# A second PSUM bank for the down sums, a fourth early expert visit, a late table in two parts, and a reordered start, in a fused attention and two-layer MoE kernel

## The reference, cut to what matters

```python
# 1. linear attention with decay: batch 4, heads 8, sequence 768, head size 48
for t in range(S):
    cur = einsum('bhd,bhe->bhde', u[None] * kt, vt)
    y[:, :, t] = einsum('bhd,bhde->bhe', rt, state + cur)
    state = wt[:, :, :, None] * state + einsum('bhd,bhe->bhde', kt, vt)
# 2. gated layer on 3072 tokens of 384 (d_ff 1024)
x = (((x @ w1) * (x @ w2)) @ w3) @ w_out
# 3. top-2 of 8 experts, noisy gate, expert d_ff 1024
noisy = x @ w_gate + log1p(exp(x @ w_noise)) * noise
top2, weights = two largest of noisy, softmax of the two
out[token] += weight * (relu(x[token] @ ew1[e]) @ ew2[e])
```

## Time and profile before

| | us |
|---|---|
| median of 3 runs | 1050.75 (1049.59, 1050.75, 1053.85) |
| the profiled execution's own time | 1053.97 |
| its span, first to last instruction | 1052.2 |
| PE busy | 1013.2 (96% of the span) |
| DVE / ACT / POOL busy | 705.6 / 584.3 / 221.7 |
| DMA | 166.41 MB, mean 158 GB/s |

### The profile page before, as it was taken

The page is one execution under the profiler, slowest core; times in us unless marked ns, Lnnn a source line. Parts: engine busy times, 40 slices in busy tenths (PEclk is TensorE's granted clock), DMA queues, the critical chain, the costliest instruction groups (busy, mean ns, idle before and its releaser), DMA issues.

```text
span 1052.2 us, 20504 instructions
## 1 busy us (share of the span) xinstructions
PE 1013.2 (96%) x7769; PEld 951.2 (90%) x7769; DVE 705.6 (67%) x1339; ACT 584.3 (56%) x1126; POOL 221.7 (21%) x210
## 2 busy tenths in 40 slices
PE   5999999999999989999998999999999999999995
PEld 3666799989999989999998999999999999999995
DVE  4789567788778767735677567575765857476570
ACT  4555446546556536533473556575665756567471
POOL 0000000110110110111313332443333234333421
PEclk9999999999999999999999999999999999999998
DMA  9564432453544542120657979787887978778761
GB/s 258 148 157 109 104 68 63 86 127 67 77 86 110 96 45 44 43 87 16 231 93 125 283 202 301 208 262 219 240 256 217 300 212 247 245 225 269 226 158 16
DMA packets 190887, 166.41 MB, mean 158 GB/s; under 512 B 118259, under 2 KB 174453, under 8 KB 190789
## 3 DMA queue, kind: packets, MB, share of 16 engines
q1 hardware_dynamic: 177012, 144.76, 49.9%
q0 software_dynamic: 12976, 20.32, 9.8%
q10 hardware_dynamic: 800, 0.02, 0.0%
HBM read 141.21 MB, written 25.22 MB: 158 GB/s over the span
## 4 chain that ended last, share of the span: by engine, by line
PE 90%; DVE 4%; ACT 2%; SPq 2%; issue 1%; DMA 0%; POOL 0%; another core or an unknown queue 0%; DVEq 0%; ACTq 0%; POOLq 0%
PE pp L1222 19%; PE bank L1206 19%; PE bank L797 19%; PE fx L813 9%; PE tr L162 3%; PE yu L1265 3%; PE fx L695 2%; PE pp L177 2%; PE yu L223 2%; PE bank L695 2%; PE yu L217 2%; PE tr L1187 2%; PE yu L1247 1%; PE fx L1247 1%; PE yu L198 1%
## 5 line engine op out<-in xcount | busy, mean ns | idle before, releaser
L797 PE MATMUL bank<-xh,w12h 128*128 128x256 f32 x576 | 167.8, 291 | 1.7 <-DVE ab_all L875 1.1
L797 PE MATMUL bank<-xl,w12h 128*128 128x256 f32 x576 | 163.5, 284 | 0.0
L797 PE MATMUL bank<-xh,w12l 128*128 128x256 f32 x576 | 163.4, 284 | 0.0
L1120 POOL DMA_INDIRECT result<-x2s,who x55 | 93.4, 1699 | 276.2 <-ACT x2s L1339 260.7
L1326 DVE SCALAR_TENSOR_TENSOR abl<-bank,abh 128x512 fp32r<-128x512 f32 x96 | 66.2, 690 | 110.7 <-ACT abh L1321 101.6
L975 POOL DMA_INDIRECT slot_entry<-entry,slot_i x48 | 48.4, 1009 | 377.3 <-DVE token_f L964 366.1
L797 PEld LDWEIGHTS bank<-xh,w12h 128*128 128x128 f32 x576 | 110.8, 192 | 4.5 <-DVE ab_all L875 2.0
L797 PEld LDWEIGHTS bank<-xl,w12h 128*128 128x128 f32 x576 | 110.9, 193 | 0.0
L797 PEld LDWEIGHTS bank<-xh,w12l 128*128 128x128 f32 x576 | 110.8, 192 | 0.0
L1206 PE MATMUL bank<-xh,set_up_h 128*128 128x256 f32 x384 | 109.2, 284 | 0.0
L1206 PE MATMUL bank<-xl,set_up_h 128*128 128x256 f32 x384 | 108.6, 283 | 0.0
(11 more groups left out here) (237 smaller groups left out, 2750.2 us busy)
## 6 DMA issues: line engine op xcount, KB each, us to landing
up_raw<-in_moe_w SPq DMA_DIRECT2D x93, 512.0 KB
down_raw<-in_moe_w SPq DMA_DIRECT2D x124, 384.0 KB
padded<-in_w SPq DMA_DIRECT2D x32, 144.0 KB, 3.1
padded<-in_k SPq DMA_DIRECT2D x32, 144.0 KB
padded<-in_r SPq DMA_DIRECT2D x32, 144.0 KB
vs<-in_v SPq DMA_DIRECT2D x32, 144.0 KB, 3.1
attention_out<-yt SPq DMA_DIRECT2D x64, 72.0 KB, 1.9
xr<-attention_out SPq DMA_DIRECT2D x12, 384.0 KB, 3.7
```

Of the source, the lines that this page charges most:

```text
L797: last = nc.tensor.matmul(bank[f % 2][:, m * TG:(m + 1) * TG], wp[:, m, kk, f * P:(f + 1) * P], xp[:, kk, :], start=(n == 0), stop=(n == 3 ...
L1120: nc.gpsimd.indirect_dma_start(out, bass.IndirectOffsetOnAxis(who[v % 4][:, s, 0:1], 0), yo[v % 2][:, s, 0:DM], None, bounds_check=N - 1, ...
```

## The change

1. `pair_slots` takes `first`: while pair 0 runs, the `diag` steps of pair 1 stand in slots 3, 4 and 5 instead of 0, 1 and 4, its `spread` steps in 6, 7, 8, 9 instead of 5, 6, 8, 9. The turns of `w_out`, the gates and the first turn of `w3` are dealt over the slots before pair 0 alone (`front`); everything from the first `w3_mm` on comes from pair 0 on. A half of the next `w3_turn` stands behind the second and fourth quarter instead of ahead of the first and third. The split of `w1`, `w2` is one block later. SP loads `w3` block 1 ahead of the second pair's w, k, r, and `w1` piece 0 behind them.
2. `pe_down` sums the second half in `bank[1]`; it waits for `fx_free` only ahead of the first half. `up` step 1 of the next group (and `hidden` step 1 of visit 0) waits for the copy out of `bank[1]`.
3. The last `place` goes to `fx` and no longer waits for `h_free`.
4. `EARLY` is 4 and `BIG` is 20; the small visits stay 5, 9, ..., 29. The late table is made in two parts: 16 instructions where all 26 stood, and the last 10 between the two `lower` halves of visit 1.
5. In the middle SP waits, after each store of `x2s`, each zeroing of `result` and each load of `xr`, until that DMA has landed, before it goes on.

```diff
-EARLY, BIG, SMALL = 3, 21, 7
+EARLY, BIG, SMALL = 4, 20, 7
...
-            for part, at in enumerate(SPREAD_AT[q]):
+            for part, at in enumerate((3, 4, 5) if first else (0, 1, 4)):
+                slots[at].append(("diag", q + 1, part))
+            for part, at in enumerate((6, 7, 8, 9) if first else SPREAD_AT[q]):
                 slots[at].append(("spread", q + 1, part))
...
             for n in range(KF):
                 for quarter in range(4):
-                    if quarter % 2 == 0 and n + 1 < KF:
+                    build.append(("w3_mm", n, quarter))
+                    if quarter % 2 and n + 1 < KF:
                         build.append(("w3_turn", n + 1, quarter // 2))
-                    build.append(("w3_mm", n, quarter))
-            order = threaded(build, first_slots() + [slot for q in range(HP) for slot in pair_slots(q)] + [[]] * TAIL)
+            order = threaded(front, first_slots())
+            order += threaded(build, [slot for q in range(HP) for slot in pair_slots(q, q == 0)] + [[]] * TAIL)
...
-                load_w12(0)
+                load_w3(1)
                 for n in range(3):
                     sp_input_load(sp, 0, 1, n)
-                load_w3(1)
+                load_w12(0)
...
-                if f == 1 and i == 0:
-                    pe.wait_ge(wal_ready, KF)
+                if f == 1:
+                    need(pe, fx_free, 2 * i)
+                    if i == 0:
+                        pe.wait_ge(wal_ready, KF)
...
-                if third == 0:
+                if third == 0 and s == 0:
                     need(pe, fx_free, fx_down(b, q, s))
...
-                        last = nc.tensor.matmul(fx[:, 0:WA], xp[:, f, s * P:(s + 1) * P], wp[:, f, :],
+                        last = nc.tensor.matmul(sum_at[s][:, 0:WA], xp[:, f, s * P:(s + 1) * P], wp[:, f, :],
...
                 if i == NG * B - 1:
-                    pe.wait_ge(h_free, 3)
+                    pe.wait_ge(fx_free, 2 * NG * B - 1)
...
+                    if j == 1:
+                        finale.append(("late", 1, 1))
                     finale.append(("lower", j, 1))
...
                             sp_group_store(sp, b, q)
+                            sp.wait_ge(x2_stored[q], 16 * (b + 1))
                         elif (step, q, n) == ("down", NG - 1, 3):
                             sp.wait_ge(fx_free, fx_down(b, q, 0) + 1)
                             sp_group_load(sp, b + 1, NG - 1)
+                            sp.wait_ge(xr_loaded[NG - 1], 16 * (b + 2))
...
                                 sp_clear(sp, HP * b + q)
+                                sp.wait_ge(zeros_stored, 16 * (HP * b + q + 1))
```

More of the change, by code:

```diff
@@ L362, in program, with pair_slots @@
         SPREAD_AT = ((5, 6, 8, 9), (5, 7, 8, 9), (5, 6, 7, 9), (6, 7, 8, 9))
[L364 to L367 removed]
+        def pair_slots(q, first=False):
+            slots = [[("score", q, 0), ("keys", q, 0)],
+                     [("score", q, 1), ("state", q, 0)],
                      [("in", q + 1, 0), ("scale", q, 0)],
                      [("in", q + 1, 1), ("derive", q + 1, 0)],
[L370 removed]
+                     [("out", q, 0), ("derive", q + 1, 1)],
                      [("out", q, 1), ("in", q + 1, 2), ("derive", q + 1, 2)],
                      [("derive", q + 1, 3)], [("derive", q + 1, 4), ("derive", q + 1, 5)], [], []]
[L373 removed]
+            for part, at in enumerate((3, 4, 5) if first else (0, 1, 4)):
+                slots[at].append(("diag", q + 1, part))
+            for part, at in enumerate((6, 7, 8, 9) if first else SPREAD_AT[q]):
                 slots[at].append(("spread", q + 1, part))
@@ L544, in first_sp @@
                         load_w3(q + 2)
-                    elif step == "w3_mm" and n == 3 and q + 2 < 6:
-                        load_w12(q + 2)
+                    elif step == "w3_mm" and n == 3 and 1 <= q < 2 * KD - 1:
+                        load_w12(q + 1)
                     elif step == "score" or step == "in" and q:
@@ L588, in first_act @@
                         evacuate(6 + 2 * q + n)
[L589 to L593, removed]
+                    elif step == "w3_mm" and n == 1 and 1 <= q <= 2 * KD:
+                        m, kk = divmod(q - 1, KD)
+                        act.wait_ge(wraw_loaded[(q - 1) % 2], 16 * ((q - 1) // 2 + 1))
+                        nc.scalar.copy(w12h[:, m, kk, :], wraw[(q - 1) % 2][:, :]).then_inc(w12h_ready, 1)
                     elif step == "w3_mm" and n == 3:
@@ L635, in first_dve @@
                                               ).then_inc(wo_ready, 1)
[L636 to L640, removed]
+                    elif step == "w3_mm" and n == 2 and 1 <= q <= 2 * KD:
+                        m, kk = divmod(q - 1, KD)
+                        dve.wait_ge(w12h_ready, q)
+                        nc.vector.tensor_tensor(w12l[:, m, kk, :], wraw[(q - 1) % 2][:, :], w12h[:, m, kk, :].bitcast(f32),
                                                 ALU.subtract).then_inc(w12l_ready, 1)
@@ L755, in fx_down, with place_at @@
                 return 2 * i + s
-            place_at = bank[0][:, 0:ST * E]
+            sum_at = (fx, bank[1])
+            def place_at(i):
+                return (fx if i == NG * B - 1 else bank[0])[:, 0:ST * E]
             CLEARS = HP * (B - 1)
@@ L852, in act_down @@
                     act.wait_ge(fx_full, fx_down(b, q, s) + 1)
-                    nc.scalar.copy(x2s[q][:, s, :], fx[:, 0:WA]).then_inc(fx_free, 1)
+                    nc.scalar.copy(x2s[q][:, s, :], sum_at[s][:, 0:WA]).then_inc(fx_free, 1)
             def act_route(act, b, q, part):
@@ L1045, in program @@
             GROUPS = NG * B
-            small = [v >= EARLY and (v - EARLY) % 4 == 2 for v in range(NV)]
+            small = [v >= EARLY and (v - EARLY) % 4 == 1 for v in range(NV)]
             slot = [BIG + sum(small[:v]) if small[v] else v - EARLY - sum(small[:v]) for v in range(NV)]
@@ L1197, in pe_hidden @@
                         pe.wait_ge(ab_free, KF * GROUPS)
-                if v < 2 and m == 0:
-                    pe.wait_ge(place_free, GROUPS - 1 + v)
+                if v == 0 and m == 0:
+                    pe.wait_ge(place_free, GROUPS - 1)
+                if v == 0 and m == 1:
+                    pe.wait_ge(fx_free, 2 * GROUPS)
                 need(pe, h_free, 4 * bigs(v) + m - 1)
@@ L1471, in rest_sp @@
                 sp_group_store(sp, B - 1, 2)
-                sp_weights(sp, 2)
+                for v in range(2, EARLY):
+                    sp_weights(sp, v)
                 for v in range(EARLY, NV):
@@ L1618, in rest_pe @@
                         pe_count(pe, GROUPS - NG)
-                    elif step == "late":
+                    elif step == "late" and n == 0:
                         pe_count(pe, GROUPS)
```

78 lines of the change are left out of this document (41 added, 37 removed).

## The result

The changed kernel takes 1046.2 us (median of 20 runs, 1038.4 to 1052.7); the kernel before, in the same comparison, 1053.3 us (20 runs, 1047.7 to 1055.6). The ratio is 0.9945, 95% interval 0.9929 to 0.9961, a gain of 5.8 us (the medians differ by 7.1). The forecast was 1037.9 us with a range up to 1043.0, so the result lies outside. In two later comparisons, in which the kernel before took 1063.1 and 1056.4 us, the changed kernel stood at 0.9945 (0.9918 to 0.9972) and 0.9992 (0.9965 to 1.0019).

A forecast was written before the change was run, and what follows sets the result against it. PE work is 90% of the chain of waits, so only closing PE holes or raising its clock saves time. 6.8 + 4.3 + 0.6 + 0 + 4.4 = 16.1 us off 1053.97 gives 1037.9 us; range 1033.4 to 1043.0.

The forecast's parts named there:

- Part 1: At the start: first scores come 9.95 us earlier, 3.13 us of work still owed; gain 6.8 us, bounds 4.0 to 7.3.
- the 18.9 us that I took: At the start: time of the first scores after the change, straight behind the gates and waiting for DVE alone.
- Parts 2 and 3: Second bank ends eight waits for the copy out of fx, 4.3 us; last place starts earlier, 0.6 us.
- Part 4: Fourth early visit, late table in two, around visit 1's hidden: gain 0; 2.5 us if ACT's lateness was chance.
- over 10 us to spare: Slack claimed for visit 4's gather, though SP reads that visit's table some 3 us later than before.
- the 1.81 us for which DVE waited for ACT: At visit 1's first hidden step, behind the late table: taken to show that removing the table alone brings nothing.
- Part 5: In the middle: SP's waits for landings remove a 3.4 us hole and 1.0 us of slow clock; 4.4 us, bounds 0 to 5.1.
- my first rival: In the middle: slow mixture stays, part 5 brings nothing, parts 1 to 3 work; 1042.3 us, chance 0.22.
- the 3.2 us between the profiled execution and the median: Whole kernel: the median lies 3.2 us below the profiled execution, whose stall was read as occurring only in some executions.
- 12.9 us: Whole kernel: forecast gain counted from the median instead of the profiled execution, 1.2%.
- some 13: End of the kernel: time without PE work behind the last matmul, in us, which the change does not touch.

The follow-up runs named there:

- e12: Kernel before with part 1 of the change alone; ratio to the kernel before 0.9931 (0.9907 to 0.9956).
- e17: Kernel before with parts 2 and 3 of the change alone; 1046.5 against 1051.4 us, ratio 0.9956 (0.9940 to 0.9972).
- e3: Kernel before with part 5 of the change alone; ratio to the kernel before 0.9997 (0.9976 to 1.0019).
- e9: The changed kernel itself, timed again in a later comparison; ratio to the kernel before 0.9945 (0.9918 to 0.9972).
- e13: The changed kernel itself, timed again in another later comparison; ratio to the kernel before 0.9992 (0.9965 to 1.0019).
- e15: Changed kernel without part 4, timed beside the changed kernel on one chip; ratio to the kernel before 0.9937 (0.9911 to 0.9964).
- e7: Changed kernel without part 4 (three early visits, late table in one piece); ratio to the kernel before 0.9879 (0.9842 to 0.9916).
- e11: Changed kernel without part 4, third visit's gather moved ahead of the last group's scatters; ratio to the kernel before 0.9889 (0.9856 to 0.9921).
- e16: Changed kernel with the third visit's gather ahead of the last group's scatters, beside the changed kernel on one chip; ratio to before 0.9839 (0.9815 to 0.9863).
- e1: Changed kernel without part 5's four SP waits; ratio to the kernel before 0.9933 (0.9908 to 0.9958).
- e2: Changed kernel, each group's x2s store held until the scatters of all groups before it have landed; ratio to the kernel before 0.9938 (0.9916 to 0.9960).
- e5: Changed kernel with the third visit's gather ahead of the last group's scatters; 1040.0 against 1057.1 us before, ratio 0.9829 (0.9804 to 0.9854).
- e18: Changed kernel with the edits of e2 and e5 together; 1033.0 us, ratio to the kernel before 0.9826 (0.9806 to 0.9845).
- e14: Changed kernel, fourth visit's weights held until the third visit's gather has landed; ratio to the kernel before 0.9941 (0.9914 to 0.9969).
- e4: Changed kernel without part 5's SP waits, each store held until earlier groups' scatters have landed; ratio to the kernel before 0.9929 (0.9908 to 0.9951).

## Why the prediction was wrong, by its own steps

**Part 1, forecast 6.8 us: right.** The first `up` came at 107.75 where 107.5 was forecast (106.6 to 110.2 over all profiles with part 1), and e12 measured 7.3 us (interval 4.7 to 9.8) at the end of the kernel. The clock stayed at 1.00 up to the first `up`. The scores were 1.2 us later than the 18.9 us that I took, for the load of `r` (1.1 us) and for DVE (0.4 us).

**Parts 2 and 3, forecast 4.9 us: right.** The waits for `x2s` are gone, none appeared at `up`, the last `place` waits 0.4 us, and e17 measured 4.6 us (2.9 to 6.3).

**Part 4, forecast 0: the step that failed.** I wrote: "Weights of visit 3 come some 4 us earlier; the PE has no hole there, so nothing." There was no hole because two ways were level: PE's own, with 2.5 us of waiting for DVE in it, and POOL's, from the scatter to the gather. In the profile before, POOL issues the second gather instruction at 569.60 us, and PE reaches the transposes 8.1 us later without a wait; the same gather took 7.9 us to land in e3 (part 5 alone), where PE waited 2.3 us for it, and 7.4 us in e17, where it waited 0.4. The slack was a microsecond or less, by this estimate. The change shortened PE's way (no wait for DVE, no wait ahead of `place`) and lengthened the other (weights beside the gather). Behind the last `place`, the third visit came after 27.1 to 28.2 us in e9 and e13, against 20.7 before. In the profile after it is 24.3: the scatter of the last group but one landed 2.1 us sooner than in e13, and POOL and the gather took 1.8 us less; the 4.0 us that PE lost there only hid the wait.

On one chip part 4 costs 5.8 us, of which the profiles of e13 and e15 show 3.9 in the third stretch and 1.7, the slower clock, in the fourth. That is about what is missing: parts 1 to 3 measured alone add up to 7.3 + 4.6 = 11.9 us, and the change gives 5.8 (0.8 in the comparison of e13). But the sum does not close in every comparison. Without part 4 the change gave 12.8 us in e7 and, with the gather first, 11.8 in e11, yet 6.7 in e15, beside which the 5.8 were measured; with part 4 and the gather first it gave 17.0 us there (e16).

I had checked the gather for visit 4 ("over 10 us to spare") but not the one for visit 2, the third, which POOL issues behind the last scatter.

Part of the 5.2 us that e15 lacks may be PE's own way; this is argued from single profiles. The 20.7 us of the profile before, on which I built, look like a favourable case: PE stands for DVE there for 2.5 us and the clock stays at 1.00. In e12, with 2.5 us of the same wait, it falls. Windows of PE, before, then e12 (columns as Rows 4):

```profile
572.00:576.00 4.00, 3.01 (x23) 2.81 (x24) 2.77 (x4) 2.62 (x5) 3.06 (x2) 1.00 1.11 90
```

```profile
572.00:576.00 4.00, 3.19 (x15) 3.20 (x16) 3.65 (x4) 2.49 (x4) 1.16 (x1) 0.50 0.92 59
```

So the wait that part 4 removes can cost more than its length, and the third stretch is 3.5 us longer in e12 than before. How often each happens in the kernel before, no run shows.

The 0 was also too low on the other side. With the gather out of the way, part 4 looks like a gain of some 5 us: 0.9829 and 0.9839 with it, 0.9889 without (e11). These are three comparisons, and the same kernel moves by as much between two of them, so the size is not shown; that PE then loses its 3.7 to 4.1 us wait for DVE (e15, e11, against 0.3 in e16) is. I had said that taking the table away alone brings nothing. I had leaned on the 1.81 us for which DVE waited for ACT behind the table. In e15 DVE goes on without it, and PE waits 3.7 us for DVE alone. Timeline of DVE, e15:

```profile
563.10 0.17 DVE L1454 CAST late_block<-block_j 128x28 int32<-128x28 f32 x1
563.19 0.68 DVE L1338 SCALAR_TENSOR_TENSOR abl<-bank,abh 128x512 fp32r<-128x512 f32 x1
```

**Part 5, forecast 4.4 us: wrong.** e3 measured nothing (0.9997, at most 2.5 us), and e1, without part 5, stood at 0.9933 where the change with it had 0.9945. Holes without a named releaser still come in the middle with all landings waited for: after has one of 6.4 us. So my first rival, that the slow mixture stays, came true, with 0.22, and by itself would have given 1042.3, which is inside the range; it took part 4 to leave it. The Trainium skill (DMA: Bandwidth & Descriptors, "Queues, rings and completion order") says that each DMA engine takes turns between queue rows packet by packet. I had read from it that holding one row back frees nobody; on the size of part 5 the runs agree, but a store held back until the scatter has landed does land sooner (2.9 against 9.1 us in e2).

**The median, and a misreading.** I took the 3.2 us between the profiled execution and the median as a stall that part 5 would remove. It was spread that both kernels have (before 1047.7 to 1055.6, after 1038.4 to 1052.7), so 12.9 us was no fair figure for the medians either; parts 1 to 3 without loss, 11.7 us by the forecast, would have given 1041.6 against 1053.3. With the gather first the changed kernel reached 1040.0, 1039.1 and 1033.0 us (e5, e16, e18), beside kernels before of 1057.1, 1056.4 and 1051.4; that this is near the forecast's 1037.9 is no merit of its sum, which held no price for the gather. One reading was off without entering the sum: behind the last matmul lie 11.8 us, not some 13.

## What to carry to other kernels

A resource without a wait in the profile may be level with the bound, not idle. Before an edit that makes PE earlier at some place, follow the other chain that ends there (here landing, scatter, gather, landing: 547.65 to 576.29 us in the profile after) and count its slack, and take a second profile if there is one. A transfer that may start earlier is an edit of its own: ask what small, awaited transfer then runs beside it; and put a gather that depends on old data ahead of the queue's newer work. One profile is one draw: the same kernel's third stretch came out at 24.3 and at 28.2 us.

## What the runs showed of the hardware that I had not expected

A scatter of 8-byte rows issued by POOL lands late: 11.5, 13.6 and 14.8 us after the start of the last of its four instructions in the chains of after, e13 and e14. What is issued right behind it starts slowly here. DMA queues of e2 in 556 to 558 us, just behind the last scatter: packets, MB, share of 16 engines:

```profile
q1 hardware_dynamic: 15, 0.06, 142.4%
q0 software_dynamic: 32, 0.00, 1.3%
```

Fifteen packets of 4 KB took 142% of 16 engines for 2 us, 3.0 us each. Ten microseconds later (566 to 568 us), beside the gather's packets, it is 0.15 us each:

```profile
q1 hardware_dynamic: 142, 0.52, 66.0%
q0 software_dynamic: 67, 0.21, 29.9%
```

The same holds for instruction loads. In the profile after, 228 to 230 us, 1.5 us and more behind the last scatter instruction of a group and with a store of `x2s` beside it, against 574 to 576 us of e2:

```profile
q8 instruction: 1, 0.02, 14.9%
```

```profile
q8 instruction: 1, 0.02, 3.3%
```

That is 4.8 us for one packet of 16 KB against 1.1 us. What the engines do at that time (ACT and PE in the profile after):

```profile
229.57 0.37 ACT L852 COPY a_sb<-bank 128x256 f32<-128x256 f32 x1 [3.24 <-issue]
237.75 0.80 ACT L232 COPY wt<-tr 128x768 f32<-128x768 f32 x1 [7.50 <-remote]
238.66 1.14 PEld L162 LDWEIGHTS tr<-ident,padded 128*128 128x128 f32 x6 [6.54 <-issue]
238.69 1.51 PE L162 MATMUL tr<-ident,padded 128*128 128x128 f32 x6 [6.36 <-ACT wt L232]
```

ACT stands for 7.5 us, though PE had ended the transposes that it copies at 230.2 us. The Trainium skill (Runtime: NRT & Kernel Launch, "Instruction fetch mechanics") says that an engine's instruction memory is refilled in blocks of 16 KiB and that the cost of crossing one is mostly hidden. Here it is not, if these loads are the cause: that ACT waited for its instructions fits the times but is argued, not shown. No run took the scatter itself away, so that it is the scatter that slows its neighbours rests on the order of events and on e2 and e4, whose stores land sooner once it is done. e2 and e18, in which the store no longer ran beside the scatters, show fewer such holes, but no gain in time that could be told from the spread. Where the run-to-run spread comes from stays open.
